# Turns rounded straight from the matmul bank: theta weights scaled at their split, and two transfers of the next phase moved back

## The chip, the cores and the metric
The kernel runs on one core of a Trainium2 chip. The metric is the time of the program on the device, in microseconds (us), lower being better. Before the change the median of three runs was 1239.06 us (1238.74 to 1240.35). For what follows, PE is the tensor engine, DVE the vector engine, ACT the scalar engine, POOL is GpSimd and SP is SyncE, which issues the transfers (DMAs).

## The reference
Everything is float32, for a batch of 8 with 576 tokens. Three layers follow each other:

```
kv  = einsum('bhsd,bhse->bhde', k, v);  out = einsum('bhsd,bhde->bhse', q, kv)
x   = (out / sqrt(mean(out*out, -1) + 1e-6)) * g_norm        # [8, 576, 512]

theta = x @ w_theta                                           # [8, 576, 512]
y   = w_tok_r @ (x * cos(theta)) + w_tok_i @ (x * sin(theta)) # over tokens, per batch
u   = x + y;   x2 = u + relu(u @ w_ch)

h   = relu(x2^T @ w_tok1) @ w_tok2;   u2 = x2 + h^T
out = u2 + relu(u2 @ w_ch1) @ w_ch2
```

The change is in `theta` and its sine and cosine, and in the order of transfers at the start of the third layer.

## The kernel before
The program has four phases, A to D. Phase A is the attention and the second layer, batch by batch (b = 0 to 7); batch 0 and batch 7 are written out, batches 1 to 6 are one loop. Phase B is the third layer's mixing over tokens (n = 0 to 7, written out). Phases C and D are the two large products. Each engine has its own instruction stream, in the order in which the code is written, and all ordering across engines is by counted semaphores; nothing is scheduled by a tool.

Matmuls in full precision are done as three: every operand is held as a "hi" part, rounded to the tensor engine's fast type, and a "lo" part, the rest (`split_matmul`, L40 to L44: lines L42, L43 and L44 are its three products). The hi parts are made by ACT, the lo parts by DVE or POOL.

In phase A a batch's 576 tokens are four chunks of 128 (j = 0 to 3) and a left chunk of 64 (j = 4). For each chunk:
- PE computes theta into a PSUM bank (`theta`, L277). Chunks 0 and 2 share one bank, 1 and 3 another, so chunk j waits until chunk j-2 has been read.
- ACT copies the bank to SBUF with the factor 1/(2 pi) (`turn`, L450; operation on L455): the angle in turns.
- DVE (`fraction`, L619) rounds the turns to a whole number by adding and subtracting 1.5 * 2^23 (L630), and subtracts that from the turns (L633). `magnitude` (L640) clears the sign bit of the fraction.
- ACT takes the sine of the fraction and the cosine from the magnitude (`sines`, L466 and L468).
- DVE multiplies both by x (`rotate`, L648 and L650).
- ACT makes the hi parts of the two products (`z_hi`, L478 and L479), POOL the lo parts (`z_lo`, L815 and L817).

The left chunk's theta is computed as two halves of the bank's partitions; ACT copies the upper half to partitions 0 to 63 and DVE adds the lower (L624).

PE mixes over tokens in `token_mix_first_half` (L306), in nine steps i, and waits at every second step: step 0 waits for the parts of chunk 0, step 2 for chunk 1, step 4 for chunk 2, step 6 for chunk 3, step 8 for the left chunk. Between theta and this mixing PE has the next batch's `kv` to do (about 5 us), except in batch 7, where there is no next batch.

In phase B, PE computes `hidden(n)` from the turned copy of x2 (x2 with the tokens on the partitions), then `mix(n)` with a part mt = 0 and a part mt = 1. The turned copy is loaded by `load_tokens(n)` (L914, DMAs on L921 and L923), split by ACT (`x_hi`, L1049) and DVE (`x_lo`), and for batches 1 and up all loads use one buffer, so `load_tokens(n)` waits for `x_lo(n-1)`. ACT has `x_hi(n+1, 0)` between the two halves of `hidden_hi(n)`, and DVE has `x_lo(n+1, 0)` between the two halves of `hidden_lo(n)`, so PE's part mt = 1 of batch n stands behind the tokens of batch n+1. `load(i, n)` (L906, L912) brings x2 itself, for the sum `residual(n)` (L1123) on DVE. Batch 7's turned x2 is written by `store_last_turned(c)` for its four column chunks c, four DMAs each (L159). The SP stream runs these in program order, each wait stopping all that stands behind it.

## Time and profile before

| | |
|---|---|
| median of three runs | 1239.06 us |
| the profiled execution, its time | 1236.66 us |
| its span, first to last instruction | 1234.5 us |
| PE busy, weight loads busy | 1190.4 us (96%), 1152.8 us (93%) |
| DVE, ACT, POOL busy | 826.6 us (67%), 504.1 us (41%), 370.5 us (30%) |
| mean granted clock of PE | 0.995 of full speed |
| DMA, mean rate over the span | 185 GB/s |

The profiled execution took 1236.66 us: 2.2 us more than its span, and 2.4 us less than the median of the timed runs. Phase A ends at about 570 us of the span, phase B runs to about 692 us. Batch 4, from which many of the rows below are, has its theta from 314 us on and its mixing from 332 us on; the loop's batches are 68.6 us apart. "Busy" of PE counts pipelined matmuls with modelled ends, so it says that PE rarely stands still, not that it is at its peak. In rows of the timeline, "x3" is the number of instructions merged in a row, and the bracket holds the idle time of the engine ahead of the row and the one that released it, by the profile; where several semaphores are waited for, the name in the bracket is the one that came last by the profile, and may be wrong.

### The profile page before, as it was taken

How to read it: one execution, taken by the hardware profiler on the slowest of the kernel's cores; microseconds unless marked ns; L12 is line 12 of the kernel's file. 1: busy time of each engine (PE TensorE's matmuls, PEld its weight loads, DVE VectorE, ACT ScalarE, POOL GpSimd, SP SyncE). 2: the span in 40 equal slices, each digit the busy share in tenths (PEclk: the TensorE clock that was granted, in tenths of full speed). 3: DMA queues.
4: the chain of work that ended last, by engine and by line, in shares of the span. 5: the costliest groups of instructions: out<-in, count | busy, mean ns of one | idle time of the engine just before them, and what ended most of it. 6: DMA issues, size and time to landing. Idle time of an engine off the chain costs nothing.

```text
span 1234.5 us, 20588 instructions
## 1 busy us (share of the span) xinstructions
PE 1190.4 (96%) x7590; PEld 1152.8 (93%) x7590; DVE 826.6 (67%) x1220; ACT 504.1 (41%) x796; POOL 370.5 (30%) x216
## 2 busy tenths in 40 slices
PE   6999999999999999979899999999999999999998
PEld 5899999989899999979798999999999899999998
DVE  3877767676867667666556477676666676666664
ACT  3633324242524334242343345555555543333331
POOL 4542535444343525340444142033112420000000
PEclk9999999999999999999999999999999999999999
DMA  9934445272533450135998677857659999999973
GB/s 249 177 56 98 78 100 91 53 139 38 125 66 76 76 114 1 47 72 172 319 325 290 202 284 269 288 206 281 249 202 336 368 322 285 277 238 308 274 190 52
DMA packets 348428, 228.12 MB, mean 185 GB/s; under 512 B 268880, under 2 KB 316368, under 8 KB 347344
## 3 DMA queue, kind: packets, MB, share of 16 engines
q1 hardware_dynamic: 348368, 227.32, 64.0%
q8 instruction: 38, 0.62, 0.2%
q14 instruction: 22, 0.18, 0.0%
HBM read 136.84 MB, written 92.80 MB: 186 GB/s over the span
## 4 chain that ended last, share of the span: by engine, by line
PE 75%; DVE 9%; issue 4%; DMA 4%; SPq 4%; ACT 4%; POOL 0%; DVEq 0%; ACTq 0%; POOLq 0%
PE bank L42 15%; PE bank L44 14%; PE bank L43 14%; PE bank L1232 9%; PE bank L1233 9%; PE bank L1234 9%; PE bank L260 3%; DVE tokens_sin L650 2%; PE bank L274 1%; DVE weights_fraction L633 1%; DMA weights_down<-w_scratch 1%; SPq L159 1%; PE bank L248 1%; DMA weights_raw_u<-u_scratch 1%; SPq L169 1%
## 5 line engine op out<-in xcount | busy, mean ns | idle before, releaser
L42 PE MATMUL bank<-weights_tok,z_z 128*128 128x288 f32 x576 | 174.4, 303 | 12.0 <-ACT z_z L479 8.8
L43 PE MATMUL bank<-weights_tok,z_z 128*128 128x288 f32 x576 | 170.4, 296 | 0.0
L44 PE MATMUL bank<-weights_tok,z_z 128*128 128x288 f32 x576 | 170.4, 296 | 0.0
L42 PEld LDWEIGHTS bank<-weights_tok,z_z 128*128 128x128 f32 x576 | 108.8, 189 | 15.6 <-ACT z_z L479 10.4
L43 PEld LDWEIGHTS bank<-weights_tok,z_z 128*128 128x128 f32 x576 | 108.8, 189 | 0.0
L44 PEld LDWEIGHTS bank<-weights_tok,z_z 128*128 128x128 f32 x576 | 108.7, 189 | 0.0
L800 POOL TENSOR_TENSOR weights_rms_inverse<-weights_mean_squares,weights_minus_half 128x8 f32<-128x8 f32 x40 | 65.5, 1639 | 135.8 <-DVE weights_mean_squares L598 135.6
L486 ACT ACTIVATE weights_x_channel_major<-attention_u 128x288 fp32r<-128x288 f32 x64 | 28.4, 444 | 148.2 <-DVE attention_u L662 148.2
L815 POOL TENSOR_TENSOR z_z<-tokens_cos,z_z 128x512 fp32r<-128x512 f32 x24 | 36.7, 1529 | 170.6 <-ACT z_z L479 170.6
L42 PE MATMUL bank<-weights_x_channel_major,weights_ch 128*128 128x288 f32 x256 | 77.2, 301 | 0.0
L43 PE MATMUL bank<-weights_x_channel_major,weights_ch 128*128 128x288 f32 x256 | 75.4, 294 | 0.0
L44 PE MATMUL bank<-weights_x_channel_major,weights_ch 128*128 128x288 f32 x256 | 75.4, 294 | 0.0
L660 DVE TENSOR_TENSOR attention_u<-bank,weights_x_channel_major 128x288 f32<-128x288 f32 x64 | 29.1, 455 | 66.3 <-PE bank L44 65.9
L1232 PE MATMUL bank<-z_u_slot,weights_up 128*128 128x384 f32 x192 | 64.5, 336 | 2.6 <-ACT bank L1472 2.0
L1459 ACT ACTIVATE attention_staged<-bank 128x384 f32<-128x384 f32 x108 | 52.3, 489 | 30.0 <-PE bank L1234 29.2
L1234 PE MATMUL bank<-z_u_slot,weights_up 128*128 128x384 f32 x192 | 64.2, 334 | 0.0
L1233 PE MATMUL bank<-z_u_slot,weights_up 128*128 128x384 f32 x192 | 64.1, 334 | 0.0
L448 ACT ACTIVATE weights_x_channel_major<-bank 128x512 fp32r<-128x512 f32 (+1 forms) x40 | 21.6, 558 | 78.0 <-PE bank L274 78.0
L808 POOL TENSOR_TENSOR tokens_x_token_major<-attention_x_normed,weights_g_norm 128x512 f32<-128x512 f32 x40 | 53.0, 1334 | 0.0
L42 PE MATMUL bank<-weights_theta,weights_x_channel_major 128*128 128x512 f32 x128 | 50.9, 398 | 0.4 <-DVE weights_theta L698 0.4
L1512 DVE TENSOR_TENSOR attention_staged<-attention_staged 128x384 f32<-128x384 f32 x36 | 33.0, 917 | 27.0 <-ACT attention_staged L1459 26.9
L44 PE MATMUL bank<-weights_theta,weights_x_channel_major 128*128 128x512 f32 x128 | 50.0, 390 | 0.0
(285 smaller groups left out, 3729.8 us busy)
## 6 DMA issues: line engine op xcount, KB each, us to landing
g_scratch<-attention_staged SPq DMA_DIRECT2D x36, 960.0 KB, 4.3
weights_g<-g_scratch SPq DMA_DIRECT2D x24, 1152.0 KB, 8.8
g_scratch<-attention_staged SPq DMA_DIRECT2D x36, 384.0 KB, 4.8
x_scratch<-attention_u SPq DMA_DIRECT2D x8, 1152.0 KB, 4.5
u_scratch<-attention_u SPq DMA_DIRECT2D x8, 1152.0 KB, 6.4
weights_raw_u<-u_scratch SPq DMA_DIRECT2D x6, 1536.0 KB, 7.8
qkv_u_left<-u_scratch SPq DMA_DIRECT2D x12, 768.0 KB, 10.1
qkv_k<-in_k_dram SPq DMA_DIRECT2D x32, 256.0 KB, 4.9
```

The costliest lines, as they stand in the source:

```text
L42: eng.matmul(out, w[0], x[0], start=first, stop=False)
L43: eng.matmul(out, w[0], x[1], start=False, stop=False)
L44: return eng.matmul(out, w[1], x[0], start=False, stop=last)
L260: mm = pe.matmul(ps_out[j % 2][:, hp * P:(hp + 1) * P], qt[:, j % 2, hp, :], kvbd[:, hp, :], start=True, stop=True)
L800: gp.tensor_tensor(rms_inv[:, i, :], msq[:, i, :], minus_half[:, :], ALU.pow).then_inc(g_pow, 1)
L808: gp.tensor_tensor(xtm[:, j, :].rearrange("p (h e) -> p h e", h=H), xn[:, i, :].rearrange("p (h e) -> p h e", h=H), gn[:, :].unsqueeze(1). ...
L815: gp.tensor_tensor(z[1][:, j, :], cos_tile[j][:, :], z[0][:, j, :].bitcast(F32), ALU.subtract).then_inc(g_zlo, 1)
L1232: eng.matmul(out, w[0], x[0], start=False, stop=False, skip_group_check=True)
L1233: eng.matmul(out, w[0], x[1], start=False, stop=False, skip_group_check=True)
L1234: return eng.matmul(out, w[1], x[0], start=False, stop=last, skip_group_check=True)
L1459: act.activation(tile(n, k), src, ACT.Relu).then_inc(done, 1)
L1512: dve.tensor_tensor(tile(n, SHARED), tile(n, LATE), tile(n, FIRST), ALU.subtract).then_inc(d_t1, 1)
```

## The change
Theta's weights are multiplied by 1/(2 pi) when they are split, so that PE's bank holds turns and no longer radians. DVE's rounding and subtracting for chunks 0 to 3 read that bank directly; ACT's copy of these chunks is gone, and `turn` becomes `turn_left`, for the left chunk alone, which now stands behind the sines of chunk 3. PE's waits for the reuse of a bank are now for DVE's subtraction (`d_frac`) and no longer for ACT's copy (`a_turns`). The lo part of the theta weights is made by a scaled subtraction. In phase B's SP stream the load of x2 of batch 1 stands behind the store of batch 0's u2, and the store of turned chunk 1 of batch 7 behind the x2 load of batch 2.

```diff
@@ PE: theta, token_mix_first_half
-                pe.wait_ge(a_turns, NT * b + j - 1)
+                pe.wait_ge(d_frac, NT * b + j - 1)
...
-            pe.wait_ge(a_turns, NT * b + NJ)
+            pe.wait_ge(d_frac, NT * b + NJ)
@@ ACT
-        def turn(b, j):
-
-            m, first = rows(j), (0 if j < NJ else LEFT)
-            act.wait_ge(p_theta, NT * b + j + 1)
-            wait(act, a_sin, 2 * (NT * b + max(j - 1, 0)))
-            act.activation(frac[0:m, j % 2, :], ps_theta[j][first:first + m, :], ACT.Copy,
-                           scale=1.0 / TWO_PI).then_inc(a_turns, 1)
+        def turn_left(b):
+            act.wait_ge(p_theta, NT * (b + 1))
+            act.wait_ge(a_sin, 2 * (NT * b + NJ - 1))
+            act.activation(frac[0:LEFT, NJ % 2, :], ps_theta[NJ][LEFT:P, :], ACT.Copy).then_inc(a_turns, 1)
...
-            act.activation(wth[0][:, cs, :], raw_theta[:, cs, :], ACT.Copy).then_inc(a_whi, 1)
+            act.activation(wth[0][:, cs, :], raw_theta[:, cs, :], ACT.Copy, scale=1.0 / TWO_PI).then_inc(a_whi, 1)
...
                 for j in range(NT + 2):
-                    if j < NT:
-                        turn(b, j)
                     if j == 2:
                         z_hi(b, 0)
                     if 1 <= j <= NT:
                         sines(b, j - 1)
+                    if j == NJ:
+                        turn_left(b)
                     if j >= 3:
                         z_hi(b, j - 2)
@@ DVE: fraction
-            dve.wait_ge(a_turns, NT * b + j + 1)
-            if j == NJ:
-                dve.scalar_tensor_tensor(out=frac[0:m, i, :], in0=ps_theta[j][0:m, :], scalar=1.0 / TWO_PI,
-                                         in1=frac[0:m, i, :], op0=ALU.mult, op1=ALU.add).then_inc(d_turns, 1)
+            turns = ps_theta[j] if j < NJ else frac[:, i, :]
+            if j < NJ:
+                dve.wait_ge(p_theta, NT * b + j + 1)
+                wait(dve, a_sin, 2 * (NT * b + max(j - 1, 0)))
+            else:
+                dve.wait_ge(a_turns, b + 1)
+                dve.tensor_tensor(turns[0:m, :], ps_theta[j][0:m, :], turns[0:m, :], ALU.add).then_inc(d_turns, 1)
                 dve.wait_ge(d_turns, b + 1)
...
-            dve.tensor_scalar(cos_tile[j][0:m, :], frac[0:m, i, :], ROUND, ROUND, ALU.add,
+            dve.tensor_scalar(cos_tile[j][0:m, :], turns[0:m, :], ROUND, ROUND, ALU.add,
                               ALU.subtract).then_inc(d_round, 1)
             dve.wait_ge(d_round, NT * b + j + 1)
-            dve.tensor_tensor(frac[0:m, i, :], frac[0:m, i, :], cos_tile[j][0:m, :],
+            dve.tensor_tensor(frac[0:m, i, :], turns[0:m, :], cos_tile[j][0:m, :],
                               ALU.subtract).then_inc(d_frac, 1)
@@ SP: load_second, sync of phase B
         load_tokens(sp, 1)
-        load(sp, 1, 1)
...
         store_last_turned(sp, 0)
-        store_last_turned(sp, 1)
...
             if n == 0:
+                load(sp, 1, 1)
                 sp.wait_ge(*prev["d_x2"])
                 load_quarter(sp, 1, 0)
                 load_quarter(sp, 1, 1)
             if n + 2 < B:
                 load(sp, n % 2, n + 2)
+            if n == 0:
+                store_last_turned(sp, 1)
             if n == 1:
                 store_last_turned(sp, 2)
```

DVE's stream in the loop of phase A, chunks 0 and 1, before the change (bank6 and bank7 hold theta, `fraction` the angle in turns and then its fraction):

```order
L630 TENSOR_SCALAR tokens0_cos_0<-weights0_fraction_0 128x512
L633 TENSOR_TENSOR weights0_fraction_0<-weights0_fraction_0,tokens0_cos_0 128x512
L640 TENSOR_SCALAR tokens0_cos_0<-weights0_fraction_0 128x512
L630 TENSOR_SCALAR tokens0_cos_0<-weights0_fraction_0 128x512
L633 TENSOR_TENSOR weights0_fraction_0<-weights0_fraction_0,tokens0_cos_0 128x512
L640 TENSOR_SCALAR tokens0_cos_0<-weights0_fraction_0 128x512
```

and after it:

```order
L631 TENSOR_SCALAR tokens0_cos_0<-bank6 128x512
L634 TENSOR_TENSOR weights0_fraction_0<-bank6,tokens0_cos_0 128x512
L641 TENSOR_SCALAR tokens0_cos_0<-weights0_fraction_0 128x512
L631 TENSOR_SCALAR tokens0_cos_0<-bank7 128x512
L634 TENSOR_TENSOR weights0_fraction_0<-bank7,tokens0_cos_0 128x512
L641 TENSOR_SCALAR tokens0_cos_0<-weights0_fraction_0 128x512
```

The instructions and their order are the same; the first two of each chunk now read the bank.

ACT's stream in the same loop, from the first chunk to the sines of chunk 1 (before the change; L455 is `turn`, L466 and L468 `sines`, L478 and L479 `z_hi`):

```order
L455 ACTIVATE weights0_fraction_0<-bank6 128x512
L455 ACTIVATE weights0_fraction_0<-bank7 128x512
L466 ACTIVATE tokens0_sin_0<-weights0_fraction_0 128x512
L468 ACTIVATE tokens0_cos_0<-tokens0_cos_0,weights0_half_pi_0 128x512
L455 ACTIVATE weights0_fraction_0<-bank6 128x512
L478 ACTIVATE z1_z_0<-tokens0_cos_0 128x512
L479 ACTIVATE z1_z_0<-tokens0_sin_0 128x512
L466 ACTIVATE tokens0_sin_0<-weights0_fraction_0 128x512
L468 ACTIVATE tokens0_cos_0<-tokens0_cos_0,weights0_half_pi_0 128x512
```

and after it (L463 and L465 are `sines`, L475 and L476 `z_hi`):

```order
L463 ACTIVATE tokens0_sin_0<-weights0_fraction_0 128x512
L465 ACTIVATE tokens0_cos_0<-tokens0_cos_0,weights0_half_pi_0 128x512
L475 ACTIVATE z1_z_0<-tokens0_cos_0 128x512
L476 ACTIVATE z1_z_0<-tokens0_sin_0 128x512
L463 ACTIVATE tokens0_sin_0<-weights0_fraction_0 128x512
L465 ACTIVATE tokens0_cos_0<-tokens0_cos_0,weights0_half_pi_0 128x512
```

The copies of the banks are gone; what remains stands in the same order.

SP's stream at the start of phase B, before the change (`z_x` is x2 of batch 1, `x_turned_last` the turned x2 of batch 7, `qkv_x_tokens` a load of tokens, `raw_up` a quarter of w_ch1, `attention_x` x2 of batch 2 here):

```order
L921 DMA qkv_x_tokens<-x_tokens_scratch 128x4x512
L923 DMA qkv_x_tokens<-x_tokens_scratch 64x512 x2
L912 DMA z_x_1_0<-x_scratch 128x1152 x2
L185 DMA x_scratch<-attention_u 128x2304
L159 DMA x_tokens_scratch<-z_x_turned_last_0 32x18x32 x4
L159 DMA x_tokens_scratch<-attention_x_turned_last_0 32x18x32 x4
L921 DMA qkv_x_tokens<-x_tokens_scratch 128x4x512
L923 DMA qkv_x_tokens<-x_tokens_scratch 64x512 x2
L964 DMA u_scratch<-attention_u_0 512x1x576
L930 DMA weights_raw_up_0<-in_moe_w_ch_dram 128x2x768 x2
L912 DMA attention_x_0_0<-x_scratch 128x1152 x2
L921 DMA qkv_x_tokens<-x_tokens_scratch 128x4x512
```

and after it:

```order
L923 DMA qkv_x_tokens<-x_tokens_scratch 128x4x512
L925 DMA qkv_x_tokens<-x_tokens_scratch 64x512 x2
L185 DMA x_scratch<-attention_u 128x2304
L159 DMA x_tokens_scratch<-z_x_turned_last_0 32x18x32 x4
L923 DMA qkv_x_tokens<-x_tokens_scratch 128x4x512
L925 DMA qkv_x_tokens<-x_tokens_scratch 64x512 x2
L964 DMA u_scratch<-attention_u_0 512x1x576
L914 DMA z_x_1_0<-x_scratch 128x1152 x2
L932 DMA weights_raw_up_0<-in_moe_w_ch_dram 128x2x768 x2
L914 DMA attention_x_0_0<-x_scratch 128x1152 x2
L159 DMA x_tokens_scratch<-attention_x_turned_last_0 32x18x32 x4
L923 DMA qkv_x_tokens<-x_tokens_scratch 128x4x512
```

Two loads of `z_x` have moved behind the store of u2, and four stores of turned chunk 1 behind the load of `attention_x`.

## Rows read from the trace of the kernel before

**Rows 1.** Timeline, tensor engine, batch 4: start us, us, engine, line, operation [idle before <-releaser].
```profile
339.04 0.37 PE L42 MATMUL bank<-weights_tok,z_z 128*128 128x288 f32 x1 [0.73 <-ACT z_z L479]
...
342.44 0.37 PE L42 MATMUL bank<-weights_tok,z_z 128*128 128x288 f32 x1
```

**Rows 2.** Chain of waits, batch 4: start us, us, what.
```profile
339.40 0.13 PE bank L43
...
342.80 0.13 PE bank L43
```

**Rows 3.** Timeline, GpSimd, batch 4.
```profile
324.63 1.42 POOL L815 TENSOR_TENSOR z_z<-tokens_cos,z_z 128x512 fp32r<-128x512 f32 x1 [18.30 <-ACT z_z L479]
326.01 1.73 POOL L817 TENSOR_TENSOR z_z<-tokens_sin,z_z 128x512 fp32r<-128x512 f32 x1
329.55 1.40 POOL L815 TENSOR_TENSOR z_z<-tokens_cos,z_z 128x512 fp32r<-128x512 f32 x1 [1.81 <-ACT z_z L479]
...
334.50 1.76 POOL L815 TENSOR_TENSOR z_z<-tokens_cos,z_z 128x512 fp32r<-128x512 f32 x1 [1.87 <-ACT z_z L479]
336.23 2.66 POOL L817 TENSOR_TENSOR z_z<-tokens_sin,z_z 128x512 fp32r<-128x512 f32 x1
...
340.55 1.75 POOL L817 TENSOR_TENSOR z_z<-attention_x_normed,z_z 128x512 fp32r<-128x512 f32 x1
```

**Rows 4.** Timeline, GpSimd, batch 1.
```profile
130.43 2.66 POOL L817 TENSOR_TENSOR z_z<-tokens_sin,z_z 128x512 fp32r<-128x512 f32 x1
```

**Rows 5.** Timeline, vector engine, batch 4.
```profile
320.49 0.43 DVE L630 TENSOR_SCALAR tokens_cos<-weights_fraction 128x512 f32<-128x512 f32 x1 [0.86 <-ACT weights_fraction L455]
...
322.62 0.69 DVE L650 TENSOR_TENSOR tokens_sin<-tokens_sin,tokens_x_token_major 128x512 f32<-128x512 f32 x1
...
324.48 0.43 DVE L640 TENSOR_SCALAR tokens_cos<-weights_fraction 128x512 int32<-128x512 int32 x1
325.72 0.88 DVE L648 TENSOR_TENSOR tokens_cos<-tokens_cos,tokens_x_token_major 128x512 f32<-128x512 f32 x1 [0.81 <-ACT tokens_cos L468]
326.53 1.76 DVE L650 TENSOR_TENSOR tokens_sin<-tokens_sin,tokens_x_token_major 128x512 f32<-128x512 f32 x1
...
335.14 1.40 DVE L640 TENSOR_SCALAR tokens_cos<-weights_fraction 64x512 int32<-64x512 int32 x1
336.47 0.68 DVE L648 TENSOR_TENSOR attention_x_normed<-attention_x_normed,tokens_x_token_major 128x512 f32<-128x512 f32 x1
...
341.16 0.42 DVE L587 COPY attention_kv_blockdiag<-bank 64x256 f32<-64x256 f32 x1
```

**Rows 6.** Timeline, scalar engine, batch 4.
```profile
319.86 0.60 ACT L455 ACTIVATE weights_fraction<-bank 128x512 f32<-128x512 f32 x1 [2.04 <-PE bank L44]
...
323.94 0.62 ACT L479 ACTIVATE z_z<-tokens_sin 128x512 fp32r<-128x512 f32 x1
```

**Rows 7.** Timeline, tensor engine, last batch of phase A.
```profile
545.88 0.37 PE L42 MATMUL bank<-weights_tok,z_z 128*128 128x288 f32 x1 [4.33 <-ACT z_z L479]
```

**Rows 8.** Timeline, SyncE (SPq), start of phase B.
```profile
583.60 8.17 SPq L159 DMA_DIRECT2D x_tokens_scratch<-z_x_turned_last  x4
591.82 5.22 SPq L159 DMA_DIRECT2D x_tokens_scratch<-ttention_x_turned_last  x4
597.08 0.53 SPq L921 DMA_DIRECT2D qkv_x_tokens<-x_tokens_scratch  x1
```

**Rows 9.** Timeline, scalar engine, start of phase B.
```profile
605.18 1.06 ACT L1049 ACTIVATE tokens_x_token_major<-qkv_x_tokens 128x1024 fp32r<-128x1024 f32 x1 [3.29 <-DMA qkv_x_tokens<-x_tokens_scratch]
...
618.93 1.05 ACT L1049 ACTIVATE tokens_x_token_major<-qkv_x_tokens 128x1024 fp32r<-128x1024 f32 x1
```

**Rows 10.** Timeline, tensor engine, start of phase B.
```profile
608.24 0.58 PE L42 MATMUL bank<-qkv_tok,z_hidden_tok 128*128 128x288 f32 x1 [2.78 <-DVE z_hidden_tok L1110]
```

**Rows 11.** Windows: stretch us, busy us of each engine, PEclk, DMA share, GB/s.
```profile
608.00:610.00 2.00, 1.76 (x7) 1.79 (x8) 1.94 (x4) 0.19 (x1) 0.00 (x0) 0.50 1.04 419
600.00:620.00 20.00, 17.22 (x90) 15.40 (x89) 8.46 (x14) 6.64 (x8) 7.49 (x3) 0.91 1.03 371
```

**Rows 12.** Timeline, vector engine, start of phase B.
```profile
592.79 0.69 DVE L1098 TENSOR_TENSOR tokens_x_token_major<-qkv_x_tokens,tokens_x_token_major 64x512 fp32r<-64x512 f32 x1
```

More of the change, by code:

```diff
@@ L530, in body @@
                         x_hi(0, j + 1)
-                    turn(0, j)
+                    if j == NJ:
+                        turn_left(0)
                     tok_weight_hi(NT + 1 + j)
@@ L552, in body @@
                         sines(b, j - 1)
+                    if j == NJ:
+                        turn_left(b)
                     if j >= 3:
@@ L697, in theta_weight_lo @@
             dve.wait_ge(a_whi, half + 1)
-            dve.tensor_tensor(wth[1][:, cs, :], raw_theta[:, cs, :], wth[0][:, cs, :].bitcast(F32),
-                              ALU.subtract).then_inc(d_wlo, 1)
+            dve.scalar_tensor_tensor(out=wth[1][:, cs, :], in0=raw_theta[:, cs, :], scalar=1.0 / TWO_PI,
+                                     in1=wth[0][:, cs, :].bitcast(F32), op0=ALU.mult,
+                                     op1=ALU.subtract).then_inc(d_wlo, 1)
         dve.wait_ge(s_zero, 6)
```

## The prediction
> **What bounds the kernel now.** I read the table of busy times first: PE is busy 96% of the span, so only what makes PE wait, or lowers its clock, can move the time. Then the waits of PE by stage, then the timelines of the four engines side by side in one batch of the loop (batch 4), where the reader is to see who really releases PE, and last the windows, for the clock and the transfers.
>
> In batch 4 PE stands still once in its mixing, 0.73 us before the product at 339.04 [rows 1]. The bracket names ACT. But that is step 4, which needs chunk 2's parts, and POOL's last one of chunk 2 runs from 336.23 for 2.66 us, to 338.89 [rows 3]: POOL is the releaser. Behind such a wait the first product takes 0.37 us where the next is 0.13 [rows 1, 2], so 0.24 us more is lost there, and 0.24 us again at 342.44 (step 6), where POOL ends at 340.55 + 1.75 = 342.30 [rows 3]. Together 1.2 us in each of the loop's six batches. Batch 7 has no other work for PE and waits 4.33 us [rows 7]. In phase B PE waits 2.78 us [rows 10] since ACT waited 3.29 us for the tokens of batch 2 [rows 9]; behind it the clock is 0.50 of full speed, the level of 1.2 GHz, and over 600 to 620 the mean is 0.91 [rows 11]: 0.09 x 20 = 1.8 us lost. I take 1.7.
>
> **The change, part by part.** *ACT's copy of a bank goes, DVE reads the bank.* Chunk 1 shows it. Before, ACT's copy starts at 319.86, DVE's rounding at 320.49 [rows 5, 6]. Now DVE starts at 319.88, 0.61 earlier, but the rounding reads PSUM. No row has this form. Below, it can't be faster than from SBUF, 0.43 [rows 5]; above, the longest rounding-like row is 1.40, one that waited [rows 5]. The nearest is the copy of 64x256 from a bank, 0.42 for half the elements; 256 more at the pace of 0.26 us per 256 (a two-input operation over 512 elements takes 0.68 [rows 5]) make 0.68. I take 0.68, 0.25 more per chunk. The subtraction already had two inputs: nothing. So chunk 0's second product (L650), at 322.62 before [rows 5], comes 0.61 - 0.25 = 0.36 earlier. The copies themselves (four of 0.60 us [rows 6]) are worth nothing more: ACT waited 2.04 us before one.
>
> The Trainium skill, "VectorE: DVE Perf Modes", Rules for kernel authors, says to accept the slow mode or copy PSUM to SBUF first where many operations follow; it gives 120 + 512 cycles for this read, an estimated 0.66 us. It speaks against the change, and with 0.66 the sum would be the same as with 0.68.
>
> *Who gets in first, POOL or DVE.* In rows 3 and 5, DVE operations with their inputs in SBUF and POOL's never run together: L640 waits for POOL's 334.50 + 1.76 = 336.26 and ends 0.28 later at 336.54; L650 at 326.53 takes 1.76, ending 0.55 behind POOL's 327.74. Before, in chunk 2, L640 at 324.48 was 0.15 ahead of POOL's 324.63 [rows 3, 5]. POOL starts 2.01 after L650 of chunk 0. L640 stood 1.86 after it and will stand 1.86 + 0.25 = 2.11 after it. So POOL is now first by 0.10: it runs from 324.27 to 325.55 (1.28 unhindered: 1.42 less the wait for L640), and L640 ends at 325.83. This is just the arrangement at 335.14: L640 waits behind one POOL operation, the next POOL operation (336.23) is already issued, and yet L648 at 336.47 takes 0.68, unhindered, and POOL's takes 2.66, waiting for two DVE products [rows 3, 5]. Batch 1 has the same 2.66 [rows 4]. So chunk 1's products will pass too: L648 at 325.76, L650 at 326.37, ended at 327.05, where it was 326.53 + 1.76 = 328.29 before. That is 1.2 us, and chunk 3 repeats the arrangement: POOL's next pair starts at 329.55, 1.26 behind L650's end, and L640 follows it by 0.09. Chunk 2's parts then reach PE over 1.2 us earlier, and the wait and both slow starts go. Gain 1.2 x 6 = 7.2, bounds 0 (the passing fails) and 7.8. PE's new waits for DVE's subtraction are met: chunk 0's subtraction is over well before chunk 1's theta is, which ends at 319.86, and the later ones likewise.
>
> *Batch 7* [rows 7]. The same 1.2 and the shorter start: 1.5, bounds 0 and the 4.33. PE still waits more than 2.78, so the slow clock behind it stays. *Batch 0*: the mixing waits for POOL behind the token weights, which don't move; 0, bounds -0.7 and 0.7. *The scaled split of the weights*: the same elements on the same engines once; 0, bounds -0.2 and 0.1. The left chunk's copy stands behind the sines of chunk 3 and is done before DVE comes to it: 0.
>
> *The transfers.* SP is held 8.17 us by chunk 0's four stores and 5.22 us by chunk 1's, and issues the tokens of batch 2 at 597.08 [rows 8]. Now chunk 1's stand behind, and SP comes to this load at 591.8 and issues it when DVE has left the buffer, at 592.79 + 0.69 = 593.5 [rows 12]. From 597.08 to ACT's start at 605.18 are 8.1 us [rows 8, 9], so they are there at 601.6; ACT would take them at 605.18 - 3.29 = 601.89. The wait goes, and with it 2.78 + 1.7 = 4.5 us. What is late next are the tokens of batch 3. Before, ACT took them at 618.93 without waiting [rows 9], but the DMA share from 600 to 620 is 1.03 [rows 11]: the transfers have no room, and the same bytes stand ahead of that load after the change, x2 of batch 1 among them, with SP held by the four stores directly ahead of it. It cannot come before 618.5. ACT will be ready at 618.93 - 4.5 = 614.4. PE resumes 608.24 - 605.18 = 3.06 behind the tokens; before, with 0.5 us of slack (3.29 - 2.78), it went on at 618.93 + 3.06 + 0.5 = 622.5. With the tokens at T it resumes at T + 3.06, after standing far longer than 2.78, so the slow clock costs its 1.7 again. Net cost T + 4.76 - 622.5 = T - 617.7. T = 618.5 costs 0.8; if SP is held as it was by chunk 0's stores (8.17 for four), T is 622 and the cost 4.3. I take T = 620.4: 2.7 us lost. Below: the transfers have room after all, a gain of 4.5.
>
> *Sum:* -7.2 - 1.5 + 2.7 = -6.0. The profiled execution of 1236.66 us becomes 1230.7; the median stands 2.4 us above it, so 1233.1 us.
>
> **Rivals.**
> *Strict turns.* POOL, issued first, goes before L648. Then chunk 1's L650 ends at 328.1 (325.83, POOL 1.14 to 326.97, 0.55 to 327.5, 0.6 to 328.1) against 328.29: the loop gains nothing, batch 7 some 0.5. For it speaks that at 326.53 DVE did wait for a POOL operation issued before it [rows 3, 5]; against it, rows 4 and 5. Time: 1239.1 - 0.5 + 2.7 = 1241.3. The Trainium skill, "SBUF — State Buffer", Who interferes with whom, says that whoever issues first gets the port pair for the whole instruction; by that rule this rival would be the result, and the row at 336.47 does not agree with it.
> *The other side: SP holds the tokens of batch 3.* Place: the four stores of chunk 1, ahead of that load; price 4.3 (T = 622) and more with each us; it decides from the point where T - 617.7 exceeds what phase A gains. With phase A at 0.5 the time is 1242.9, with 7.2 + 1.5 it is not slower. For it: 8.17 [rows 8]; against: 5.22.
> *Both halves gain.* The tokens of batch 3 are early enough: 1239.1 - 8.7 - 4.5 = 1225.9. Against it: the share of 1.03 over 20 us.
> *Half a gain.* DVE's L640 is first after all (rounding under 0.58): the shift of 0.36 to 0.6 alone, 6 x 0.5 + 1 = 4.0 less 2.7: 1237.8.
> *x2 of batch 1 late.* Issued near 597 and there 8.1 later, at 605 to 607, about when DVE comes to it: 0 to 1 us, inside the other ranges, since PE stands still right after.
>
> **How the numbers follow.** Forecast 50%, strict turns 14%, the held tokens with no gain in phase A 8%, both halves gain 10%, half a gain 18%. The forecast's own range is 1229 to 1237 (phase A 5 to 8.7, phase B 0 to 4.3). The 8-in-10 range reaches to the strict turns and to part of the double gain: 1227.5 to 1241.5. A measurement of this kernel tells about 0.2%, 2.5 us, from no change: 1236.6 to 1241.5. Faster holds the forecast's most (48), both halves (10), and some half gains (7): 0.65. Same: 0.20. Slower: 0.15.
>
> **What would show it.** Right: the loop's batches 67.4 us apart and not 68.6; no idle time at PE's step 4; DVE's L640 of chunks 2 and 3 at about 1.4 us and the products of chunk 1 at 0.68 instead of 0.88 and 1.76; rounding from the bank at 0.68; PE's wait gone in batch 1 of phase B and a longer one, with the low clock behind it, in batch 2. Wrong: L650 of chunk 1 still at 1.76 (strict turns), the rounding over 0.9 us, ACT waiting for no tokens in batch 2 of phase B, or PE waiting in the loop for DVE's subtraction.

## The result, and the profile after

The changed kernel takes 1241.88 us (median; 1239.57 to 1245.95, 14 runs), the kernel before in the same job 1238.47 us (14 runs): ratio 1.0031, 95% interval 1.0021 to 1.0041. By the ratio it is slower by about 4 us (2.6 to 5.1). Forecast were 1233.1 us and faster. The profiled execution took 1240.46 us with a span of 1238.3, against 1236.66 and 1234.5.

The span is cut here at marks that both traces have: the first wait of PE in batch 0's mixing, SP's store of x2 at the end of phase A (L185), PE's first product of phase C, its first wait of about 0.58 (0.58 before, 0.56 after) in phase D.

| stretch, us | before | after | difference | forecast |
|---|---|---|---|---|
| start to batch 0's mixing | 56.99 | 56.55 | -0.44 | 0 |
| from there to the end of phase A | 526.22 | 524.11 | -2.11 | -8.7 |
| phase B | 109.45 | 110.81 | +1.36 | +2.7 |
| phase C | 263.46 | 266.94 | +3.48 | 0 |
| phase D | 278.38 | 279.89 | +1.51 | 0 |

**The loop gained nothing.** The timeline of DVE and then of POOL in batch 4, and the same wait of PE, to be held against [rows 1, 3, 5]:

```profile
322.70 0.68 DVE L631 TENSOR_SCALAR tokens_cos<-bank 128x512 f32<-128x512 f32 x1
323.42 0.69 DVE L634 TENSOR_TENSOR weights_fraction<-bank,tokens_cos 128x512 f32<-128x512 f32 x1
324.14 1.48 DVE L641 TENSOR_SCALAR tokens_cos<-weights_fraction 128x512 int32<-128x512 int32 x1
325.54 1.78 DVE L649 TENSOR_TENSOR tokens_cos<-tokens_cos,tokens_x_token_major 128x512 f32<-128x512 f32 x1
...
330.66 1.76 DVE L649 TENSOR_TENSOR tokens_cos<-tokens_cos,tokens_x_token_major 128x512 f32<-128x512 f32 x1
...
334.98 1.40 DVE L641 TENSOR_SCALAR tokens_cos<-weights_fraction 64x512 int32<-64x512 int32 x1
336.30 0.68 DVE L649 TENSOR_TENSOR attention_x_normed<-attention_x_normed,tokens_x_token_major 128x512 f32<-128x512 f32 x1
336.91 0.67 DVE L651 TENSOR_TENSOR attention_x_normed<-attention_x_normed,tokens_x_token_major 128x512 f32<-128x512 f32 x1
```
```profile
324.05 1.29 POOL L817 TENSOR_TENSOR z_z<-tokens_cos,z_z 128x512 fp32r<-128x512 f32 x1 [17.89 <-ACT z_z L476]
325.30 1.47 POOL L819 TENSOR_TENSOR z_z<-tokens_sin,z_z 128x512 fp32r<-128x512 f32 x1
...
334.35 1.75 POOL L817 TENSOR_TENSOR z_z<-tokens_cos,z_z 128x512 fp32r<-128x512 f32 x1 [2.48 <-ACT z_z L476]
336.06 2.66 POOL L819 TENSOR_TENSOR z_z<-tokens_sin,z_z 128x512 fp32r<-128x512 f32 x1
```
```profile
338.87 0.37 PE L42 MATMUL bank<-weights_tok,z_z 128*128 128x288 f32 x1 [0.72 <-ACT z_z L476]
```

DVE's rounding now reads the bank in 0.68 us, and POOL was there ahead of the magnitude of chunk 2 (L641 at 324.14 takes 1.48, behind POOL's 324.05), both as forecast. But its second subtraction, issued at 325.30, then went before the product of chunk 1 (L649 at 325.54, 1.78), and again at 330.66. At 336.30 the two products do go ahead of POOL's 336.06, as they did before [rows 3, 5]. So chunk 2's parts come no earlier, and POOL's 336.06 + 2.66 still sets PE's start at 338.87. The batches stay 68.6 us apart.

**Batch 7**: PE waits twice, 2.45 + 1.28 = 3.7 us, where it waited three times before, 4.33 [rows 7] and two of 0.74 and 1.11, 6.2 us together. The first of the two is PE's new wait for DVE's subtraction:

```profile
535.21 0.40 PE L42 MATMUL bank<-weights_tok,z_z 128*128 128x288 f32 x1 [2.45 <-DVE weights_fraction L634]
...
544.62 0.37 PE L42 MATMUL bank<-weights_tok,z_z 128*128 128x288 f32 x1 [1.28 <-ACT z_z L476]
```

**Phase B**: SP's issues, ACT's taking of tokens, PE, and the windows (busy times by engine, then PEclk, DMA share), against [rows 8 to 11]:

```profile
590.16 0.40 SPq L923 DMA_DIRECT2D qkv_x_tokens<-x_tokens_scratch  x1
...
598.67 9.19 SPq L159 DMA_DIRECT2D x_tokens_scratch<-ttention_x_turned_last  x4
607.91 1.58 SPq L923 DMA_DIRECT2D qkv_x_tokens<-x_tokens_scratch  x1
```
```profile
597.98 1.05 ACT L1052 ACTIVATE tokens_x_token_major<-qkv_x_tokens 128x1024 fp32r<-128x1024 f32 x1
...
616.22 1.06 ACT L1052 ACTIVATE tokens_x_token_major<-qkv_x_tokens 128x1024 fp32r<-128x1024 f32 x1 [5.39 <-DMA qkv_x_tokens<-x_tokens_scratch]
```
```profile
619.28 0.58 PE L42 MATMUL bank<-qkv_tok,z_hidden_tok 128*128 128x288 f32 x1 [4.88 <-DVE z_hidden_tok L1113]
```
```profile
617.00:625.00 8.00, 5.72 (x26) 5.75 (x27) 6.28 (x10) 3.60 (x5) 3.86 (x2) 0.57 1.02 322
```

The tokens of batch 2 cost no wait; those of batch 3 do, since chunk 1's four stores now hold SP for 9.19 us (5.22 before [rows 8]) right ahead of their load. Around the end of PE's 4.88 us the granted clock is 0.57 over 8 us, that is, mostly at its lower level (1.2 GHz). For the first 2.3 of these 8 us PE still stands. What it loses falls behind 619.28: to 625.00 the mean granted clock is 0.55, and 0.45 x 5.7 = 2.6 us are lost. Before, it was 0.58 from 608.24 to 612.00, and 0.42 x 3.8 = 1.6 us.

**Phase C** has a wait that nothing in the prediction speaks of. PE waits for a weight that DVE had from ACT, and ACT stood still, released by nothing; then ACT's rows at the same place before:

```profile
702.21 0.41 PE L1235 MATMUL bank<-qkv_u_slot,weights_up 128*128 128x384 f32 x1 [4.61 <-DVE qkv_u_slot L1304]
```
```profile
694.52 0.49 ACT L1485 ACTIVATE qkv_up_t<-bank 128x384 f32<-128x384 f32 x1 [0.51 <-PE bank L44]
700.23 0.84 ACT L1300 ACTIVATE qkv_u_slot<-weights_raw_u 128x768 fp32r<-128x768 f32 x1 [5.22 <-issue]
```
```profile
695.74 0.49 ACT L1482 ACTIVATE qkv_up_t<-bank 128x384 f32<-128x384 f32 x1 [0.51 <-PE bank L44]
696.12 0.84 ACT L1297 ACTIVATE qkv_u_slot<-weights_raw_u 128x768 fp32r<-128x768 f32 x1
```

### The profile page after: what moved, and what is told of

The parts are those of the page before. It is cut to its first block, busy times and chain, and to the rows that moved or that the text cites. A ratio compares the mean times of both kernels' runs of the same rounds, so it can differ in the third digit from the quotient of the medians.

```text
span 1238.3 us, 20568 instructions
## 1 busy us (share of the span) xinstructions
PE 1193.1 (96%) x7590; PEld 1156.5 (93%) x7590; DVE 842.0 (68%) x1220; ACT 489.2 (40%) x764; POOL 363.2 (29%) x216
## 4 chain that ended last, share of the span: by engine, by line
PE 67%; issue 13%; DVE 9%; POOL 3%; DMA 3%; SPq 2%; ACT 2%; DVEq 0%; POOLq 0%; ACTq 0%
PE bank L42 12%; PE bank L44 12%; PE bank L43 12%; PE bank L1235 9%; PE bank L1237 9%; PE bank L1236 9%; PE bank L260 2%; DVE tokens_cos L649 2%; DMA weights_down<-w_scratch 1%; PE bank L248 1%; POOL weights_rms_inverse L802 1%; POOL tokens_x_token_major L810 1%; DVE weights_fraction L634 1%; DMA g_scratch<-attention_staged 1%; DVE tokens_sin L651 1%
## 5 line engine op out<-in xcount | busy, mean ns | idle before, releaser
L42 PE MATMUL bank<-weights_theta,weights_x_channel_major 128*128 128x512 f32 x128 | 51.0, 398 | 0.4 <-DVE weights_theta L699 0.4
L676 DVE SCALAR_TENSOR_TENSOR attention_u<-bank,attention_u 128x288 f32<-128x288 f32 x64 | 28.3, 452 | 32.3 <-PE bank L44 32.3
```

Of the source, the lines that this page charges most:

```text
L42: eng.matmul(out, w[0], x[0], start=first, stop=False)
```

## The experiments

Each is timed against the kernel before on the same chip. The profiled executions differ by up to 3.8 us ahead of batch 0's mixing, so stretches are compared, not spans. "Loop" is the distance of two batches; where a kernel has two values, its batches take the one or the other. The last column is from batch 0's mixing to the end of phase A.

| kernel | median us | ratio to before [95%] | loop | phase B | phase C | phase A |
|---|---|---|---|---|---|---|
| before | 1237 to 1238.5 | 1 | 68.61 | 109.5 | 263.5 | 526.2 |
| after | 1241.88 | 1.0031 [1.0021, 1.0041] | 68.61 | 110.8 | 266.9 | 524.1 |
| e1 transfers only | 1241.48 | 1.0036 [1.0022, 1.0050] | 68.64 | 111.0 | 263.1 | 527.6 |
| e2 banks only | 1238.54 | 1.0008 [0.9997, 1.0020] | 68.63 | 107.6 | 267.7 | 525.5 |
| e3 after, ACT padded | 1237.18 | 0.9999 [0.9989, 1.0009] | 68.60 | 110.5 | 263.2 | 524.0 |
| e4 magnitude on 128 rows | 1243.51 | 1.0061 [1.0042, 1.0079] | 68.94 | 109.8 | 267.0 | 526.4 |
| e5 magnitude in halves | 1255.11 | 1.0148 [1.0135, 1.0162] | 69.8, 71.3 | 110.1 | 267.0 | 539.5 |
| e6 banks, padded | 1234.51 | 0.9980 [0.9969, 0.9990] | 68.61 | 108.1 | 263.4 | 525.3 |
| e7 as e6, halves | 1251.61 | 1.0113 [1.0096, 1.0129] | 69.8, 71.3 | 109.9 | 263.2 | 542.0 |
| e8 before, stores later | 1235.47 | 0.9986 [0.9977, 0.9996] | 68.63 | 106.0 | 263.2 | 527.3 |
| e9 e3 with e8's stores | 1233.09 | 0.9969 [0.9958, 0.9980] | 68.60 | 105.2 | 262.8 | 524.2 |
| e10 after, POOL yields | 1230.36 | 0.9949 [0.9936, 0.9963] | 67.39 | 110.0 | 266.8 | 515.4 |
| e11 e9 and e10 | 1224.16 | 0.9899 [0.9884, 0.9914] | 67.39 | 107.5 | 264.1 | 515.4 |
| e12 as e5, halves turned round | 1252.48 | one run | 70.0, 71.5 | 110.1 | 266.7 | 538.9 |
| e13 half, product, half | 1257.02 | one run | 70.0, 71.6 | 110.0 | 266.9 | 542.6 |
| e14 before, POOL yields | 1232.23 | 0.9951 [0.9933, 0.9969] | 67.97 | 109.9 | 264.5 | 522.4 |
| e15 e14 with e8's stores | 1229.99 | 0.9931 [0.9917, 0.9945] | 67.95 | 105.7 | 263.2 | 520.7 |

**The two halves of the change apart.** e1 is the kernel before with only the part of the diff that is in `load_second` and `sync`; e2 is all the rest.

> The kernel before with the two moves on SP alone (x2 of batch 1 behind the first store of u2, the turned chunk 1 behind the next load of x2); banks and weights as before. Theory: phase A is not touched, its end stays within 0.5 us of before; the tokens of batch 2 cost ACT no wait, those of batch 3 cost it about 5 us, PE stands about 5 us there and shows the half clock for two stretches of 3.4 us instead of one. Net the start of phase C is 1 to 2.5 us later than in the kernel before, and no wait of PE over 3 us stands in the first 20 us of phase C, since ACT's stream of instructions is the old one: 1240 us (+1.5). Rival, the prediction's bill: +2.7, 1241.2. Rival 2, the stall of ACT in phase C belongs to the moved transfers: it shows here too, with 5 us of idle time of ACT that nothing releases, and the time is 1243.

> The kernel after with SP's order of before: only the turns from the bank and the scaled weights are left of the change. Theory: the batches of the loop stay 68.6 us apart, phase A ends 1.5 to 2.5 us earlier (batch 7), phase B is as before, and if the idle time of ACT at the start of phase C comes from its shorter stream, PE waits there 4.6 us: sum -2 +3.5 = 1240. Rival: the stall belongs to the transfers, it is absent, 1236.5.

e1 costs 0.36%, no less than the whole change (0.31%); its phase B is 1.5 us longer, with PE waiting 4.99 us at 623.89. Its time is nearer to the rival's 1241.2 than to the theory's 1240. Phase C is that of before. Its phase A is 1.4 us longer with the same code and no longer wait of PE: around the end of batch 7's wait of 4.33 us the granted clock is 0.57 over the 8 us from 545 on, and was 0.57 over the 4 us from 546 on before. So this part is not shown to be the transfers' doing. e2 alone is no different from before: its phase C is 4.2 us longer, more than the 0.7 of phase A and the 1.8 of phase B that it gains (PE waits 1.88 us for the tokens of batch 2 there, and not 2.78). So the idle time of ACT comes with the banks, not with the transfers.

**ACT's idle time is its stream of instructions.** e3 has eleven small activations more, at the start, where ACT waits anyway:

```diff
+        for pad in range(11):
+            act.activation(cos_t[:, 0, pad + 1:pad + 2], half_pi[:, :], ACT.Sin, scale=0.5)
         act.activation(cos_t[:, 0, 0:1], half_pi[:, :], ACT.Sin, scale=0.5).then_inc(a_table, 1)
```

> The kernel after with 11 activations of 128x1 more in ACT's stream, at its very start where ACT is idle for 11.6 us anyway, so that all that follows in this stream stands again near where it stood before the change. Theory (code loading): ACT's 5.2 us of idle time before its first weight preparation of phase C are the loading of instructions, which falls elsewhere now; PE's wait of 4.61 us and the half clock behind it go, and the time is 3.5 to 4.6 us less than after: 1237.5 to 1238.5. Rival: the idle time is a wait for data or for a slot that the profile does not name; it stays at 5.2 us and the time is that of after, 1241.9.

They take 1.14 us together. Below them is the place of the 5.22 us:

```profile
5.31 1.14 ACT L506 ACTIVATE tokens_cos<-weights_half_pi 128x1 f32<-128x1 f32 x11 [3.29 <-POOL weights_half_pi L835]
...
697.12 0.49 ACT L1487 ACTIVATE qkv_up_t<-bank 128x384 f32<-128x384 f32 x1 [0.51 <-PE bank L44]
697.50 0.84 ACT L1302 ACTIVATE qkv_u_slot<-weights_raw_u 128x768 fp32r<-128x768 f32 x1
```

Neither the data nor the waits in the code differ from after; eleven instructions that run 690 us earlier take the stall away, and with it 3.7 us of phase C and 0.3% of the time. In all, phase C is 266.7 to 267.7 us in the seven kernels that have the short stream (the banks read by DVE, no padding) and 262.8 to 264.5 in the ten others. The trace names what ACT waits for only as "issue". But its list of transfers has a queue named "instruction" (q14). In each of the seven, 8192 bytes are loaded on it 7.0 to 7.2 us into phase C (at 698.54 after), and ACT, idle for 5.2 to 5.3 us, goes on 1.7 us behind that (at 700.23). In the ten others this queue loads nothing in the first 30 us of phase C; its last load is 12.8 to 16.9 us ahead of it. That ACT stood for its instructions fits all seventeen; only which engine this queue serves the trace doesn't say. e6 is e2 with this padding:

> Banks alone (as e2) with the 11 small activations ahead of ACT's stream (as e3). Theory: what the two have apart adds up: phase A gives about 2.2 us in batch 7, the transfers cost nothing, the stall of ACT in phase C is gone: 1235 to 1236.5, and PE waits nowhere over 4 us in phases B and C. Rival: the gain of batch 7 is given back in phase B by slack that was there anyway (PE waits for the tokens of batch 2 the longer): 1237.8, as before.

It came as the theory had it, or a little better (1235 to 1236.5 was expected): 0.20% faster than before, with a longest wait of 2.46 us in phase B.

**Who goes first.** e4 takes the magnitude of the left chunk over all 128 rows (`m` is `P` in `magnitude`).

> The kernel after, in which the magnitude of the left chunk (64 rows) is taken over all 128 rows (the other 64 rows of the tile are written over later; the output is the same). It asks why DVE's two products of chunk 3 pass a subtraction that POOL issued before them (2.66 us on POOL) while those of chunks 1 and 2 do not (1.47). Theory: a DVE operation on 64 rows ahead of them lets them pass. Then here, with 128 rows, they do not pass: POOL's second subtraction of chunk 2 takes 1.5 instead of 2.66, DVE's first product of chunk 3 takes 1.8 instead of 0.68, PE's wait of 0.73 at step 4 of each batch goes, and up to half of it comes back at step 6: the batches 68.0 to 68.6 apart, 1238.5 to 1241.9. Rival: the history of the two engines (POOL's first subtraction had itself waited 0.5 us) decides, the rows do not matter: nothing changes, 2.66 stays, 1241.9.

DVE in batch 4, and POOL:

```profile
337.28 1.40 DVE L641 TENSOR_SCALAR tokens_cos<-weights_fraction 128x512 int32<-128x512 int32 x1
338.61 1.77 DVE L649 TENSOR_TENSOR attention_x_normed<-attention_x_normed,tokens_x_token_major 128x512 f32<-128x512 f32 x1
```
```profile
338.36 1.47 POOL L819 TENSOR_TENSOR z_z<-tokens_sin,z_z 128x512 fp32r<-128x512 f32 x1
```

The magnitude takes its 1.40 as before, and yet the product behind it no longer passes: 1.77 for 0.68, 1.47 for 2.66. The rows of the magnitude decide. The time went further than expected (1238.5 to 1241.9; the batches are 68.94 apart): PE's wait moved two steps on and became 1.30 us. e5 and e7 then took chunks 2 and 3 in two halves, rows 64 to 127 first; e12 the other way round:

```diff
+            for rs in (slice(LEFT, P), slice(0, LEFT)) if j in (2, 3) and not (isinstance(b, int) and b == 0) else (slice(0, m),):
+                op = dve.tensor_scalar(cos_tile[j][rs, :].bitcast(I32), frac[rs, i, :].bitcast(I32), 0x7FFFFFFF, None,
+                                       ALU.bitwise_and)
+            op.then_inc(d_abs, 1)
```

> The kernel after, in whose batches 1 to 7 the magnitudes of chunks 2 and 3 are each taken in two operations, first rows 64 to 127, then rows 0 to 63. Run e4 showed that DVE's products pass POOL's queued subtraction behind a 64-row operation and not behind a 128-row one. Theory: the products of chunks 1 and 2 now pass as well (0.68 instead of 1.76), at the price of one more 64-row operation each (about 0.4). Chunk 2's product ends 0.8 to 1.1 us earlier than in after, POOL's second subtractions take 2.6 or more instead of 1.47, PE's wait of 0.73 at step 4 goes and the batches of the loop are 67.6 to 68.2 apart: 6 x 0.4 to 1.0 less, 1236 to 1239.5. Rival: what counts is that the left chunk's magnitude is the last of its batch, or the history of the engines; the products keep their 1.76, DVE only has 0.7 us more per batch: 1242 to 1244.

> e6 with the split magnitudes of e5. Theory (64-row operations let the products pass): 2.4 to 6 us less than e6, 1230 to 1234. Rival (the rows do not matter): 0.5 to 2 us more than e6. If e5's split changes DVE's stream so that its own loading of instructions falls into a critical place, a new wait of PE of 2 to 5 us shows which it is.

> As e5 (magnitudes of chunks 2 and 3 in two operations of 64 rows), but rows 0 to 63 first, then rows 64 to 127. In e5 POOL's second subtraction got in between the two halves. In the kernel after, DVE's products pass behind an operation on rows 0 to 63. Theory (what is queued behind an operation on rows 0 to 63 passes): here the second half passes, the two together take 1.8 instead of 2.9, and POOL's second subtraction of chunk 0 takes 1.8 or more instead of 1.48. Rival (the rows by themselves are not what lets it pass): 2.9 and 1.48 again, 1255.

The theories of all three missed, and for e5 and e7 the rivals' times too. For e12 its rival held (1252.48 us, one run):

```profile
332.64 2.91 DVE L642 TENSOR_SCALAR tokens_cos<-weights_fraction 64x512 int32<-64x512 int32 x2
```

POOL's subtraction takes 1.47 there. The second half waits for POOL too, ACT's cosine waits for both halves, and a batch costs 1.2 to 3 us more. e13 has the second half behind the products of the chunk before:

```diff
+                        magnitude(b, j, slice(0, LEFT) if split else None)
                     if j >= 1:
                         rotate(b, j - 1)
+                    if split:
+                        magnitude(b, j, slice(LEFT, P))
```

> The kernel after, in whose batches 1 to 7 the magnitude of chunks 2 and 3 is taken for rows 0 to 63 as before ahead of the products of the chunk before, and for rows 64 to 127 behind them. Theory: a full product directly behind a 64-row magnitude passes POOL's queued subtraction, as in chunk 3: the first products of chunks 1 and 2 take 0.68 instead of 1.78, POOL's second subtractions 2.6 instead of 1.47. Rival: that is not the condition either, 1.78 and 1.47 stay, and the cause stays open.

```profile
331.81 1.47 DVE L642 TENSOR_SCALAR tokens_cos<-weights_fraction 64x512 int32<-64x512 int32 x1
333.21 0.67 DVE L652 TENSOR_TENSOR tokens_cos<-tokens_cos,tokens_x_token_major 128x512 f32<-128x512 f32 x1
333.81 0.67 DVE L654 TENSOR_TENSOR tokens_sin<-tokens_sin,tokens_x_token_major 128x512 f32<-128x512 f32 x1
```
```profile
332.96 2.66 POOL L825 TENSOR_TENSOR z_z<-tokens_sin,z_z 128x512 fp32r<-128x512 f32 x1
```

Now the products of chunk 1 pass (0.67, 0.67; POOL 2.66), in each of batches 1 to 7 (POOL 2.65 to 2.67). So a full product behind a 64-row magnitude goes ahead of POOL's operation that was issued before it; behind a 128-row magnitude it does not. That POOL's first subtraction had itself waited, the rival named for e4, is not the cause: in e4 it takes 1.76 and the product does not pass, in e13 it takes 1.29, unhindered, and the product passes. As a kernel it is worse, 1257.02 us (one run): the second half comes late for ACT. The Trainium skill, "SBUF — State Buffer", Who interferes with whom, has it that the first to issue gets the shared ports. The rows at 325.54 here and at 338.61 in e4 agree; those at 336.30 here and 333.21 in e13 do not. Why the rows matter no run shows.

**What the step would have been worth.** e10 brings about by a wait what the prediction expected of the hardware: POOL's second subtraction of chunks 0 and 1 stands behind both products of the next chunk.

```diff
+                if j in (0, 1) and not (isinstance(b, int) and b == 0):
+                    gp.wait_ge(d_z, 2 * (NT * b + j + 2))
                 gp.tensor_tensor(z[1][:, NJ + j, :], sin_tile[j][:, :], z[0][:, NJ + j, :].bitcast(F32),
```

> The kernel after, with one wait more on POOL in batches 1 to 7: its second subtraction of chunk 0 is issued when DVE's first product of chunk 1 and all before it are done, that of chunk 1 likewise behind chunk 2's. It tests the step of the prediction that failed: that DVE's products go ahead of POOL's queued operation there. Theory (the step was wrong on who goes first, and right on what that is worth): the two first products take 0.68 instead of 1.78, chunk 2's parts reach PE 1.2 to 2.3 us earlier, PE's wait at step 4 and both slow starts go, the batches are 67.4 apart instead of 68.6, and batch 7 gives up to 1 more: 1233.5 to 1235.5. Rival: the next limit stands right behind (POOL's second subtraction of chunk 2, or step 6), and half or less of it is had: batches 68.0 or more, 1238 to 1241.

DVE in a batch, and windows of two batches (us, then busy time of PE, PEld, DVE, ACT, POOL):

```profile
321.93 1.48 DVE L641 TENSOR_SCALAR tokens_cos<-weights_fraction 128x512 int32<-128x512 int32 x1
323.32 0.68 DVE L649 TENSOR_TENSOR tokens_cos<-tokens_cos,tokens_x_token_major 128x512 f32<-128x512 f32 x1
...
327.40 0.68 DVE L649 TENSOR_TENSOR tokens_cos<-tokens_cos,tokens_x_token_major 128x512 f32<-128x512 f32 x1
```
```profile
321.80:389.20 67.40, 67.40 (x489) 65.16 (x488) 48.36 (x86) 23.38 (x45) 26.43 (x19) 1.00 0.45 88
389.20:456.60 67.40, 67.40 (x490) 65.16 (x489) 48.37 (x86) 23.35 (x45) 26.42 (x20) 1.00 0.44 88
```

PE is busy for 67.40 of 67.40 us: no idle time of PE is left in the loop for a better order to take away. Phase A is 8.7 us shorter than after's, and more was had than expected (0.51% under before, 0.8% under after).

> The kernel before with the waits on POOL of e10 and nothing else. Theory: the waits do in the kernel before what they do in the one after, since both have the same products at 1.76 and the same wait of PE: the batches 67.4 apart, phase A 8 us shorter, and no stall of ACT in phase C: 1228 to 1231. Rival: reading the banks is needed for it (the copies hold DVE's chain back by 0.36 a chunk): the batches 67.7 or more apart, 1231 to 1235.

The rival held (67.97 apart, 1232.23 us): with the copies of before a batch takes 67.97 instead of 67.39. Reading the bank is worth 0.58 us a batch, but only once POOL gives way.

**Why the tokens of batch 3 are late.** e8 is e1 with the stores of chunks 1, 2 and 3 one step later:

```diff
-            if n == 0:
-                store_last_turned(sp, 1)
-            if n == 1:
-                store_last_turned(sp, 2)
-            if n == 2:
-                store_last_turned(sp, 3)
+            if 1 <= n <= 3:
+                store_last_turned(sp, n)
```

> The kernel before with x2 of batch 1 loaded behind the first store of u2, as in the change, but the stores of the turned chunks 1, 2 and 3 of the last batch one step later each (behind the x2 loads of steps 1, 2 and 3). Theory: the 4.9 us that PE stands for the tokens of batch 3 in e1 are SP being held for 9 us by the four stores of chunk 1 right ahead of that load. Without them SP issues it at about 601 instead of 608, it lands before 613, and PE's waits for tokens are gone from batches 2 and 3 (under 1 us): 1233 to 1235 (4.5 less than before by the prediction's sum). Rival (the transfers themselves have no room, whatever the order): the tokens of batch 3 land at 616 or later, PE stands 4 to 5 us, 1240 to 1242.

```profile
600.67 1.01 SPq L912 DMA_DIRECT2D attention_x<-x_scratch  x2
605.91 0.38 SPq L921 DMA_DIRECT2D qkv_x_tokens<-x_tokens_scratch  x1
```
```profile
618.91 0.37 PE L42 MATMUL bank<-qkv_tok,z_hidden_tok 128*128 128x288 f32 x1 [1.51 <-DVE z_hidden_tok L1107]
```

The four stores were the cause: without them ahead, PE waits 1.51 us and phase B is 4.9 us shorter than in e1 and 3.4 shorter than before. The load is issued at 605.9 and not at 601 as expected, behind SP's wait for DVE to leave the buffer; from this comes the wait that is left, and the time, 1235.47 us, is a little over the theory's. e8 has the moved x2 load as well, so that load alone can't be what costs in e1.

**All together.**

> The kernel after with the padded stream of ACT (e3) and the stores of the turned chunks 1, 2 and 3 one step later each (e8). Theory: gains of e6 (2.4 us, batch 7) and of e8 (1.7 to 4.5 us, phase B) stand beside each other: 1230.5 to 1233.5, PE waits under 2 us in phase B. Rival: with batch 7 shorter the same transfers bound phase B, so that one of the two is lost: 1235.

> e9 and e10 together: what each gives apart adds up. By the theory 7 us under e9, 1224 to 1227; by e10's rival 1229 to 1233. If the wait on POOL moves its stream so that its loading of instructions falls into a critical place, a new wait shows.

> e14 with the order of the transfers of e8 and e11. It differs from e11 in the banks and the scaled weights alone. If reading the banks is worth nothing once POOL gives way: within 1.5 us of e11, 1223 to 1226. If it is still worth the 2.5 us of batch 7 that e6 had over before: 1226 to 1228.

The gains add up: from after, e9 takes 0.62% and e10 0.82%, both together 1.32%. e11 beats both kernels: 1224.16 us, 1.01% under before (0.86 to 1.16). e15 differs from it in the banks, the scaled weights and the padding, and is 0.3% behind; 1229.99 is more than either figure named.

## Why the prediction was wrong, by its own steps

- **"So chunk 1's products will pass too"** is the step that failed. It took -7.2 for the loop from one row, POOL's 2.66 at 336.23 [rows 3], and its repeat in batch 1 [rows 4]. The operation ahead of the product there works on 64 rows, those of chunks 1 and 2 on 128, which was legible in [rows 5]. The row of the same form, L650 at 326.53 with 1.76 behind a POOL operation, spoke the other way. Measured: 0 for the loop, the strict turns that had 14%. That this rival's time, 1241.3, is so near to the 1241.88 measured is in part luck: it has nothing of phase C's 3.5 us. e4 and e13 show the condition, e10 that the price was right: 1.2 us a batch, 67.39 where 67.4 was named, and more in batch 7.
- What led up to that step held: rounding from the bank at 0.68 (0.68 estimated), POOL first by 0.09 (0.10), the magnitude at 1.48 (1.4 to 1.5), and PE's new waits met in the loop.
- **Batch 7** was -1.5 and is -2.1 for all of phase A, with no products passing. The new wait for the subtraction (2.45 us) was not seen; fewer waits followed it. The size hangs on the clock: after, the lower level falls behind the first wait (0.57 over 535.2 to 539.2), and the second is 1.28 us; in e2, with the same code, it falls behind the second (0.57 over 547.5 to 551.5), which is 2.85 us, and phase A is 0.7 us shorter than before, in e6 0.9.
- **Phase B** was +2.7 (0.8 to 4.3), and is +1.4 in the profile and +1.5 in e1's stretch. The mechanism (SP held in front of the tokens of batch 3) is shown by e8. Two sizes were off: ACT took the tokens at 616.22, or 618.8 in before's time (2.6 us added, by which the end of phase A is earlier), against T = 620.4, 1.6 less; and the clock cost 2.6 and not 1.7, 0.9 more. By the prediction's own way of counting that makes 1.1 + 0.9 = 2.0. It is 1.8 at PE's next wait, 0.83 us in both kernels (78.5 us behind the end of phase A at 661.69 before, 80.2 at 660.90 after). A wait of 0.31 us behind it, at 672.59, is in the kernel before alone and takes the rest down to the 1.4 that were measured, to within 0.1.

  e1's whole ratio, 2.7 to 6.2 us, is wider than its stretches (2.5 us), so the bill of the transfers is known to no better than that.
- **Phase C** was 0 and is +3.5. Without it (e3) the change would have been no different from before: the sum of what was foreseen, with the failed step at 0, is -1.5 + 2.7 = +1.2 us, and e3 measured 0 (-1.4 to +1.1), so the sum stands just outside.
- **Phase D** took 278.4 us in nine of the seventeen profiled kernels and 279.9 in eight, with and without the change on either side; before is one of the first, after one of the second, and they differ at one wait:

```profile
1004.44 0.44 PE L1232 MATMUL bank<-qkv_g_hi,weights_down 128*128 128x384 f32 x1 [2.42 <-DVE bank L1811]
```
```profile
1006.67 0.69 PE L1235 MATMUL bank<-qkv_g_hi,weights_down 128*128 128x384 f32 x1 [3.66 <-DVE bank L1814]
```

  The low clock makes the two lengths. In the nine it falls 20 us behind the start of phase D (before: 0.57 over 976 to 980), ahead of this wait, which takes up part of it; in the eight it falls 48 us behind it, right after the wait (after: 0.58 over 1006 to 1010), where nothing does. The 1.5 us between the two profiles are therefore not shown to be the change's; what picks one of the two places is open.

## What to carry to other kernels

Before a rule is read out of one row, compare the operation ahead of it in engine, form and rows with the place to which it is carried. Where two engines hold each other up, as DVE and POOL do here (1.76 us for 0.68), and one of them has slack, give the order by a wait and don't leave it to who issues first: the wait on POOL gave the kernel before 0.5%, more than twice the 0.2% that the bank reads give without it (e6). A diff that shortens an engine's stream moves every later instruction of it, and here that was worth 0.3%. If an idle time released by "issue" shows up far from the change, pad the stream before looking for a cause in the data. And before a difference of 1 to 2 us between two profiles is put down to a change, see whether the low clock falls at the same place in both.

## What the runs showed that was not expected

- The two 128-row products pass a POOL operation issued 0.24 us before them when the DVE operation ahead, a magnitude, is on 64 rows (0.68 and 2.66); when it is on 128 rows the first waits 1.1 us (1.76 to 1.78, and 1.47).
- The length of phase D takes two values 1.5 us apart in 17 kernels, by where the low clock falls in it.
- ACT stood for 5.2 us for no data, over 150 us behind the last of its instructions that was changed, until 8192 bytes had been loaded on an instruction queue, and 11 instructions of 0.1 us at the start undid it.
- Four stores issued from SP hold it for 4.1 to 9.2 us (4.12 for chunk 0's in e1, 9.19 for chunk 1's after), by where they stand in its stream.
